# Gated stage of a batch cut into units between the heads of the next batch; paired k/q transposes; P normalised on GpSimd

## The reference, cut to what matters

```
# attention: B=4, H=8, S=576, D=64
scores = q @ k.T / sqrt(D)                      # per head
cum    = cumsum(max(s, 0))
scores = where(causal, -1e9, scores + min(-(cum[:,None] - cum[None,:]), 0))
P      = exp(scores - max);  P = P / (sum(P) + 1e-9);  x = P @ v
# gated stage, per batch: x is 576 x 512
h      = gelu_tanh(x @ w_in)                    # 512 x 1024
u, v   = h[:, :512], h[:, 512:]
v_n    = (v - mean) / sqrt(var + 1e-6) * g_ln
v_s    = w_sg @ v_n + b_sg                      # mixes tokens of the batch
x      = x + (u * v_s) @ w_out
# routed experts: each token goes to one of 8 experts (512 x 1024, relu, 1024 x 512)
```

## Time and profile before

| | |
|---|---|
| time, median of 3 runs | 942.02 us (939.26, 942.02, 942.26) |
| profiled execution, span | 940.1 us; its own time is not listed apart and is one of the same kind, so some 1.9 us lie around the span |
| PE busy | 873.8 us, 93% of the span |
| DVE, ACT, POOL busy | 55%, 43%, 11% |
| mean granted clock of TensorE | 0.971 of full speed |
| chain that ended last | 90% on PE |

### The profile page before, as it was taken

The page is one execution under the profiler, slowest core; times in us unless marked ns, Lnnn a source line. Parts: engine busy times, 40 slices in busy tenths (PEclk is TensorE's granted clock), DMA queues, the critical chain, the costliest instruction groups (busy, mean ns, idle before and its releaser), DMA issues.

```text
span 940.1 us, 19053 instructions
## 1 busy us (share of the span) xinstructions
PE 873.8 (93%) x5573; PEld 725.9 (77%) x5574; DVE 517.7 (55%) x1021; ACT 405.3 (43%) x990; POOL 99.3 (11%) x187
## 2 busy tenths in 40 slices
PE   4899999999999989999999999748999999999993
PEld 2677778787787769988988989546888888888773
DVE  6567767777677743624535335384556266536221
ACT  2566666666666644215134142233435244415110
POOL 0001111111111020000000000001111111111111
PEclk9999999999999989999999999858999999999997
DMA  6422232222323100001001001196345255511100
GB/s 165 146 66 66 58 70 53 67 62 58 71 52 71 39 20 1 1 1 50 0 0 50 0 0 52 57 351 224 117 147 201 77 199 205 210 49 35 38 33 21
DMA packets 100842, 74.88 MB, mean 80 GB/s; under 512 B 81416, under 2 KB 81416, under 8 KB 100778
## 3 DMA queue, kind: packets, MB, share of 16 engines
q1 hardware_dynamic: 96810, 63.21, 22.1%
q0 software_dynamic: 4000, 11.28, 3.7%
HBM read 64.43 MB, written 11.86 MB: 81 GB/s over the span
## 4 chain that ended last, share of the span: by engine, by line
PE 90%; DVE 3%; DMA 2%; SPq 2%; issue 2%; ACT 1%; POOL 0%; POOLq 0%; ACTq 0%; DVEq 0%
PE sbank L1020 24%; PE obank L728 10%; PE sbank L1611 9%; PE sbank L1613 9%; PE sbank L1612 9%; PE tbank L709 5%; PE sbank L694 5%; PE sbank L696 3%; PE obank L719 2%; PE tbank L672 2%; PE obank L1068 2%; PE tbank L677 1%; PE tbank L1596 1%; PE tbank L1636 1%; PE sbank L701 1%
## 5 line engine op out<-in xcount | busy, mean ns | idle before, releaser
L455 ACT ACTIVATE probs<-sbank,nmax 128x128 f32<-128x128 f32 (+4 forms) x160 | 90.8, 568 | 55.3 <-DVE nmax L585 55.2
L728 PE MATMUL obank<-pT,v_raw 128*64 128x128 f32 (+2 forms) x960 | 113.2, 262 | 0.3 <-ACT recipT L474 0.3
L728 PEld LDWEIGHTS obank<-pT,v_raw 128*64 128x64 f32 (+1 forms) x960 | 91.5, 136 | 11.4 <-ACT recipT L474 0.5
L585 DVE TENSOR_REDUCE nmax<-sbank 128x1 f32<-128x128 f32 (+4 forms) x160 | 86.5, 541 | 15.4 <-PE sbank L701 12.0
L694 PE MATMUL sbank<-k,q 128*128 128x256 f32 (+2 forms) x192 | 76.6, 404 | 0.8 <-ACT probs L455 0.8
L1611 PE MATMUL sbank<-w_high,xsT_h 128*128 x184 | 74.8, 407 | 2.0 <-DVE xsT_l L1536 1.7
L1120 DVE TENSOR_TENSOR w_low<-w_low,w_high (+1 forms) x64 | 74.0, 1216 | 0.7 <-ACT w_high L1476 0.3
L709 PE MATMUL tbank<-ident,probs 128*128 128x128 f32 (+2 forms) x480 | 73.9, 267 | 0.2 <-ACT probs L455 0.2
L1613 PE MATMUL sbank<-w_low,xsT_h 128*128 x184 | 72.6, 395 | 0.0
L1612 PE MATMUL sbank<-w_high,xsT_l 128*128 x184 | 72.4, 394 | 0.0
L1611 PE MATMUL sbank<-w_high,hidT_h 128*128 x176 | 70.9, 403 | 0.2
(11 more groups left out here) (230 smaller groups left out, 1983.5 us busy)
## 6 DMA issues: line engine op xcount, KB each, us to landing
w_low<-in_moe_w_dram SPq DMA_DIRECT2D x16, 2048.0 KB, 13.4
k_raw<-in_k_dram SPq DMA_DIRECT2D x64, 128.0 KB, 2.3
q_raw<-in_q_dram SPq DMA_DIRECT2D x32, 128.0 KB, 2.3
v_raw<-in_v_dram SPq DMA_DIRECT2D x32, 128.0 KB, 2.2
x_dram<-x SPq DMA_DIRECT2D x4, 1024.0 KB, 4.4
win_raw<-in_moe_w_in_dram SPq DMA_DIRECT2D x1, 2048.0 KB, 8.0
wsg_raw<-in_moe_w_sg_dram SPq DMA_DIRECT2D x1, 1152.0 KB, 6.3
k_raw<-in_k_dram SPq DMA_DIRECT2D x64, 16.0 KB, 2.1
```

The lines of the kernel that those rows point to most:

```text
L455: nc.scalar.activation(probs_view(u, i, r), score_view(i, r), ACT.Exp, bias=nmax[u][0:r, i:i + 1], accum_out=sums[u][0:r, i:i + 1]).then_i ...
L585: nc.vector.tensor_reduce(nmax[u][0:r, i:i + 1], src, ax, ALU.max, negate=True).then_inc(maxed, 1)
L728: mm = nc.tensor.matmul(obank[0:D, c, a:a + w], v_raw[u][0:r, j, :], pT[0:r, j, P * i:P * i + w], start=(j == 0), stop=(j == i))
```

## The change

- Heads are worked in pairs. Both k's of a pair stand side by side in one 128-column tile, and both q's, so one transpose turns two heads. They are made at the end of an odd slot (`pair_main`) with the 64-row tails in the even slot after it (`pair_tails`). Head u keeps its rows where the transpose puts them, and POOL writes the second copy of the high parts of k and q (`twice`).
- P is divided by its sum before its transpose: DVE inverts in three pieces (`invert`), POOL multiplies (`norms`). `turn_recips`, the widened reciprocals and their copy go. The output is a plain copy.
- The banks change: five score blocks share three banks, the fourth (`O`) takes the output and the turned q, and the two banks of `obank` are free for the gated stage.
- The gated stage of batch b is cut into 37 units of one bank each, at 32 points between the instructions of the heads t = 9+8b to 16+8b (`point_of`, `fill(t, k)`: five points in an odd slot, three in an even one; the last three points hold two, three and three units). The last batch is done behind the attention as before. The GELU of batches 0 to 2 is written out: halve (ACT), square (POOL), cube term (DVE), tanh (ACT), product (DVE).
- Slots 1 to 5 carry the transposes of w_sg, which stood ahead of the first head; slots 2 to 6 carry the split of w_in and w_out, in 8 shares (POOL high, DVE low) for 16 (ACT, DVE).
- The loops over heads and batches are written out.

```diff
+        def point_of(t, k):
+            n = t - HPB - 1
+            b, s_ = n // HPB, n % HPB
+            if n < 0 or b >= B - 1:
+                return None
+            return b, (s_ // 2) * 8 + (k if s_ % 2 == 0 else 5 + k)
...
+            def twice(p, u, cols, n):
+                pool.wait_ge(kq_high, 5 * p + n)
+                nc.gpsimd.tensor_copy(k1[u][other_rows[u], cols], k1[u][own_rows[u], cols].bitcast(F32))
+                nc.gpsimd.tensor_copy(q1[u][own_rows[u], cols],
+                                      q2[u][own_rows[u], cols].bitcast(F32)).then_inc(kq_twice, 1)
...
+                for i in range(first, end):
+                    w = probs[u][0:r, OFF_P[i]:OFF_P[i] + W_P[i]]
+                    nc.gpsimd.tensor_scalar(w, w, recip[u][0:r, i:i + 1], None, ALU.mult).then_inc(normed, 1)
...
+            for t in range(HEADS + 1):
+                this, before, even = t < HEADS, t >= 1, t % 2 == 0
+                h = t - 1
...
+                    turn_probs(h, 0, 0)
+                    turn_probs(h, 1, 0, P).then_inc(p_turned, 1)
+                if this:
+                    scores(t, 0)
+                fill(t, 0)
+                if this:
+                    scores(t, 1)
+                    if even:
+                        pair_tails(t // 2)
...
+                    turn_probs(h, 2, 1).then_inc(p_turned, 1)
+                if this:
+                    scores(t, 2)
+                fill(t, 1)
...
+                    turn_probs(h, 3, 0).then_inc(p_turned, 1)
+                if this:
+                    scores(t, 3)
...
+                    turn_probs(h, 4, 1).then_inc(p_turned, 1)
+                fill(t, 2)
+                if before:
+                    attends(h)
+                if this:
+                    scores(t, 4)
+                if not even:
+                    fill(t, 3)
+                    if t + 1 < HEADS:
+                        pair_main((t + 1) // 2)
+                    fill(t, 4)
```

More of the change, by code:

```diff
@@ L110, in moe_block @@
         aug = pr("aug", [HEADS, 2, 4, S], F32)
[L111 to L132, removed]
-        prep.close()
[L135 to L142, removed]
+        prep.close()
+        prep = ExitStack()
+        win_raw = tensors(prep)("win_raw", [P, KT, FF2], F32)
+        prep.close()
+        x_h = fb("x_h", [P, KT, SP], F32R)
+        x_l = fb("x_l", [P, KT, SP], F32R)
+        g_h = x_h
         same_place = ExitStack()
@@ L519, in _ @@
[L519 to L532 removed]
+                    exps(t, 3)
@@ L534, in _ @@
+                fill(t, 2)
+                if this:
+                    exps(t, 4)
+                if not even:
+                    fill(t, 3)
+                    if t + 1 < HEADS:
+                        pair_main((t + 1) // 2, 0)
+                    fill(t, 4)
+                    if t + 1 < HEADS:
+                        pair_main((t + 1) // 2, 1)
+                elif t >= HPB and t % HPB == 0:
+                    x_high(t // HPB - 1, 3)
         @block.vector
@@ L607, in slot, with invert @@
-            def slot(t, u, pair=None, this=True, before=True, earlier=True, after=True):
+                nc.vector.tensor_reduce(nmax[u][0:r, i:i + 1], score_view(i, r), ax, ALU.max,
+                                        negate=True).then_inc(maxed, 1)
+            def invert(t, first, end):
+                u, r = t % 2, rows_of[first]
+                n = 3 * t + first // 2 + 1
+                dve.wait_ge(exped, ST * t + end)
+                nc.vector.tensor_scalar(sums_eps[0:r, first:end], sums[u][0:r, first:end], 1e-9, None,
+                                        ALU.add).then_inc(eps_added, 1)
+                dve.wait_ge(eps_added, n)
+                nc.vector.reciprocal(recip[u][0:r, first:end], sums_eps[0:r, first:end]).then_inc(inverted, 1)
@@ L610, in slot @@
                 if before:
[L611 removed]
+                    invert(t - 1, 4, 5)
+                fill(t, 0)
                 if this:
[L613 to L619 removed]
+                    row_max(t, 1)
+                    if even:
+                        pair_tails(t // 2)
@@ new lines, in _ @@
+                    invert(t, 2, 4)
+                    row_max(t, 4)
+                if not even:
+                    fill(t, 3)
+                    if t + 1 < HEADS:
+                        pair_k((t + 1) // 2, 0)
+                        pair_q((t + 1) // 2, 0)
+                    fill(t, 4)
+                    if t + 1 < HEADS:
+                        pair_k((t + 1) // 2, 1)
+                        pair_q((t + 1) // 2, 1)
+                elif t >= HPB and t % HPB == 0:
+                    x_low(t // HPB - 1, 3)
```

1403 lines of the change are left out of this document (792 added, 611 removed).

## The result

The changed kernel takes 984.09 us (median of 4 runs, 981.49 to 985.13), the kernel before 941.36 beside it: a ratio of 1.0455, with an interval of 1.044 to 1.047. It is slower by 43 us. The prediction said 964 with 926 to 988: slower was right, and the time lies inside the range. It is 20 above the forecast and outside the 950 to 976 of the forecast case: the range reaches it because rivals 1 and 2 were in it. The profiled execution has a span of 981.8 us.

The account below looks back on a forecast made before the run. The prediction took PE as the bound nearly everywhere, with the order of waits deciding the gain. The span of 940.1 plus 14 (stage A) plus 8 (stage B) made 962, with 1.9 to the median 964 us; range 926 to 988.

Parts of the forecast that it names:

- forecast case: Whole kernel: the summed forecast of 964 us holds, 950 to 976; chance 0.40.
- rival 1: POOL's scaling and copies cost twice the copy rows, about 22 us over 15 pairs: 985 to 990; chance 0.12.
- rival 2: PE falls to its lower rate in slots without fills, 12 to 20 us more: 976 to 984; chance 0.15.
- PE's saving: Attention on PE: reciprocal transposes gone and k, q transposes paired, 1.26 us a head, 40 us over 32 heads.
- Stage A: Start of the kernel to slot 9: slot 9 starts at 128 instead of 113.5, 14 us later.
- The waits of the hand-over: Between pairs, PE waits 3.1 us for POOL's copies, 1.5 at block 4, 1.2 at the next border.
- The weights: Stage A, slots 3 to 6: weight shares add 2 us a slot, with the w_sg steps 9 to 10.
- Stage B: Slots 9 to 32 with three batches: 387 us of work and 40 of waits, 427, 8 more than before.
- The last points: Stage B, end of each batch's units: three units in two banks wait for ACT, 3 us.
- Rivals 3 and 4: rival 3, and a fourth case: the parts cancel, time within 0.3% of before; chance of that 0.06.
- rival 3: Units cover nearly all waits in stage B, which gains 22 to 31 us: 925 to 934; chance 0.27.
- Stage C: Last batch and experts behind attention: order kept, no difference, give or take 1 us.

Follow-up runs that it names:

- e3: Changed kernel with all 37 units of a batch in one piece at the start of slots 9, 17 and 25: 1049.5 us, ratio 1.118.
- e6: Kernel before, with only P scaled on POOL and the transposes of reciprocals gone: 938.5 us, ratio 0.997.
- e2: Changed kernel with POOL scaling only one column of each block of P, so P is not normalised: 968.2 us, ratio 1.030.
- e9: Changed kernel with both POOL's scaling of P and the written-out GELU narrowed to one column: 948.1 us, ratio 1.008.
- e4: Changed kernel with square, cube term, tanh and product of the written-out GELU on one column, GELU left out: 961.5 us, ratio 1.024.
- e8: e6 with, on PE, the scores of block 3 ahead of the transposes of block 2 of P: 932.2 us, ratio 0.991.
- e10: e8 with ACT copying the tails of k and q ahead of exponential 2: 919.2 us, ratio 0.977 to the kernel before.
- e1: Changed kernel with POOL's copies of the next pair's k and q ahead of the scaling of blocks 2 and 3: 979.6 us, ratio 1.043.
- e5: Changed kernel with the next pair's k and q moved ahead of the last exponential and both fills on PE, ACT, DVE and POOL: 982.9 us, ratio 1.045.
- e7: Changed kernel with ACT's own GELU in place of the written-out one for batches 0 to 2: 987.8 us, ratio 1.047.

## Why the prediction was right, and where its size was off

**PE's saving.** Right: 36 us of busy time for 40, at a mean granted clock that fell from 0.971 to 0.944. The pair's work was put too high, by 0.4 us a slot: 16.0 us at the full clock (e3) for 16.9. e6 shows what the prediction said of all such savings, that they count only if the others keep up, and sharpens it: even with every engine below PE's sum, 0.71 us of PE work can be the cover of a wait of nearly the same length.

**Stage A.** The waits of the hand-over were right (3.02, 1.50 and 1.03 for 3.1, 1.5 and 1.2), though the second came in two of four slots only; so were the first scores, 19.57 for 19.5. That the border fell at 128.1 for 128 is luck. Two terms were off and cancelled. The weights were put at 2 us a slot in waits, 9 to 10 us in all with w_sg; the waits from slot 2 to slot 8 are 19.2 us in sum, which is the pairs' own 20 and leaves nothing for the weights. In their place PE ran at its lower rate for part of these slots, which the sum had at nothing: the granted clock is 0.88, and PE is busy for 68.3 us of the 87.8, where seven slots of 8.45 and four steps of w_sg of 0.7 make 62.0. With the 8.0 a slot of e3 it is 9 us more and not 6. That is rival 2's mechanism, at about half of its size; the forecast of A came out only because the weights cost less.

**Stage B.** Here the forecast was too low: 40 us of waits and 387 of work, where 56 and 391 came. Batch 1, whose waits are 20.1 for the 13.5 of the forecast, tells which terms of the waits. The pair of slots 9 and 10 was right in sum and by luck: 2.20, 0.53 and 1.95, 4.7 in all, for 0.7, 2.1 and 1.7. The slots of mix and projection wait 1.5 where I put 4. Three terms were too small. Up to the first scores of slot 12 PE waits 7.2, where the sum of 13.5 leaves 2 besides the terms that the text names: the prediction looked at DVE's rows and ACT's table loads there, and not at POOL's, where a square, five casts and the slow scaling stand ahead of the copies. DVE was late there too: without the scaling 5.36 remain (e2). The last points are 4.2 for 3. And 2.5 for the low part of x at the first unit of slot 9 was not in the sum. DVE was to be busy for 80% of stage B; it is for 64% (286.0 of 447.5), so it was not the sum of its work. In the work two errors cancelled: the same products of PE took 382.3 us in e9 at a granted clock of 0.98, so the 387 was at least 5 too high, and the lower rate, which the sum left out, made 9 or more.

**Rival 1.** The prediction said it would be too low if 512 columns took POOL over 1 us, or if pitches of 0.42 appeared in stage B. Both came: 512 columns take POOL 1.6, and the first products of stage B start every 0.43. Of rival 1's two conditions the scaling's came true, and the copies' did not: they take 0.65, as their rows had it, so the 1.2 that rival 1 gave them stayed out. And the price was not 22: e2 puts the scaling at 10, of which 8.4 are in B. In slots 2 to 8 the scaling ends just as ACT hands q over. So the scaling explains 8 of the 20 us that were missing in B. How the rest splits between DVE's two GELU passes, ACT's exponentials and the lower rate isn't settled, since e4, e2 and e9 don't add up (22, 10, 36.6): narrowing one load uncovers the next.

**Rivals 3 and 4** fell: the units between heads cover some 6 us against a gapless gated stage (the estimate at e3), where rival 3 asked for 22 to 31 less than the kernel before. e9 shows what rival 3 needed, B under 418.6: neither load on the engines. Even then A keeps the whole at 1.008.

**Stage C** gave 1.8 us back, where the prediction had at most 1 either way.

## What to carry to other kernels

When PE work goes, look at what ran during it: here 0.71 us of transposes were the cover of a bank's copy, and the gain came only with the next independent work moved into its place, wait by wait (e6, e8, e10). Keep operands ready one whole slot ahead of their use: pairing saved an estimated 0.55 us of transposes a head and put a chain of row maximum, exponential, ACT and POOL in front of PE every second head, a wait of 3.02 us, 1.5 a slot, where nothing covered it; the waits for turned P, for POOL's scaling and for a bank added another 1.5 (e3). No run takes the pairs alone out of the changed kernel, but with k and q ready a slot ahead e10 runs without a gap. And when one wait in such a chain is shortened, expect the next one to take it (e1, e5): count the pair, not the wait. When a variant's time moves, split it into waits and busy time before naming a cause: in e7 and in e3 20 us of the difference were PE at its lower rate, and not waits.

## What the runs showed of the hardware

- A multiply by a column of factors on POOL took 1.60 us for 128x512 and 1.83 for 64x576, where copies with a cast took 0.65 for 512 columns and, in the kernel before, 0.66 for 64x576: about 2.5 and 2.8 times, on one input. The square, which reads its operand twice, took 1.04. The rule of the Trainium skill that the prediction weighed (GPSIMD Engine Reference, "Key points": the vector engine is structurally about twice as fast for elementwise work) is borne out by the scaling (a DVE pass over 512 columns, L807, took 0.76) and half by the square, not by the copies.
- PE's lower rate came behind its longest waits: after 7.18 us idle, products of 288 columns started every 0.24 us instead of 0.13. How much of a stretch ran so differs where the code is the same: 0.83, 0.88 and 0.90 of the full clock in slots 2 to 8 of e4, of the changed kernel and of e7, with PE busy for 71.4, 68.3 and 66.6 us. Beside waits it can be free: pairs of 22.1 us at 1.00 and at 0.90 (e3).
- ACT's table loads took 1.28 us each. With 63 more of them, 81 us on ACT, the kernel's time moved by no more than its scatter (e7).
